# Attention output kept transposed in SBUF through the attention stage and stored to DRAM after the last loads

## The reference

```python
# attention over memory slots, per batch and head (b = h = 8, s = 576, d = 64, m = 32)
a = softmax(phi, axis=s); k_m = einsum('bhsm,bhsd->bhmd', a, k); v_m = einsum('bhsm,bhsd->bhmd', a, v)
attn = softmax(q @ k_m.T / sqrt(d)) @ v_m
x = attn reshaped to (4608, 512)
# first layer: w_in (512, 2048), w_out (2048, 512)
h = x @ w_in; x = (h * sigmoid(1.702 * h)) @ w_out
# mixture of 8 experts, the top one of each token: w1[e] (512, 1024), w2[e] (1024, 512)
out = gate_weight * output_gate * (relu(x @ w1[e]) @ w2[e])
```

## Time and profile before

| | us |
|---|---|
| three runs | 1408.29, 1414.30, 1414.38 |
| median | 1414.3 |
| the profiled execution's own time | 1402.57 |
| its span in the profile | 1400.9 |
| mean granted clock of TensorE | 0.993 |

### The profile page before, as it was taken

The page is one execution under the profiler, slowest core; times in us unless marked ns, Lnnn a source line. Parts: engine busy times, 40 slices in busy tenths (PEclk is TensorE's granted clock), DMA queues, the critical chain, the costliest instruction groups (busy, mean ns, idle before and its releaser), DMA issues.

```text
span 1400.9 us, 26210 instructions
## 1 busy us (share of the span) xinstructions
PE 1351.8 (96%) x7922; PEld 1094.9 (78%) x7923; DVE 681.5 (49%) x1400; ACT 403.2 (29%) x725; POOL 517.7 (37%) x612
## 2 busy tenths in 40 slices
PE   5888899999999999999999999999999999999997
PEld 4566688888888888888888888887788888888885
DVE  4789633344353343433534344436655555555553
ACT  2455422222232232222322223223332222223221
POOL 1100486345443343433433334331434333433331
PEclk9999999999999999999999999999999999999999
DMA  9999635656556556465465654665784688649882
GB/s 229 290 325 313 234 100 168 194 200 194 181 191 183 179 169 182 171 187 175 160 183 176 179 192 147 184 189 203 236 257 119 164 254 249 185 115 261 246 237 61
DMA packets 164843, 275.31 MB, mean 197 GB/s; under 512 B 20179, under 2 KB 57316, under 8 KB 164788
## 3 DMA queue, kind: packets, MB, share of 16 engines
q1 hardware_dynamic: 104260, 197.16, 44.7%
q10 hardware_dynamic: 47408, 45.63, 12.7%
q0 software_dynamic: 13120, 31.82, 7.3%
HBM read 146.03 MB, written 100.45 MB: 176 GB/s over the span
## 4 chain that ended last, share of the span: by engine, by line
PE 86%; DVE 5%; DMA 3%; issue 3%; SPq 2%; ACT 0%; ACTq 0%; POOL 0%; DVEq 0%; POOLq 0%
PE ps L672 28%; PE ps L706 28%; PE ps L776 14%; PE ps L747 14%; DMA ph<-in_phi 1%; PE ps L716 1%; DMA qraw<-in_q 1%; SPq L426 1%; SPq L454 1%; PE ps L649 1%; DVE cmeta L1123 1%; DVE phT L1101 1%; DMA cq<-ch 1%; PE ps L631 0%; DMA cmeta<-record_scratch 0%
## 5 line engine op out<-in xcount | busy, mean ns | idle before, releaser
L672 PE MATMUL ps<-xs,W 128*128 (+1 forms) x1728 | 417.6, 391 | 1.1 <-DVE xs L1162 1.1
L706 PE MATMUL ps<-W,gs 128*128 128x512 f32 x1728 | 415.3, 390 | 0.1
L672 PEld LDWEIGHTS ps<-xs,W 128*128 128x128 f32 x1728 | 323.1, 188 | 72.0 <-issue 4.1
L706 PEld LDWEIGHTS ps<-W,gs 128*128 128x128 f32 x1728 | 324.3, 188 | 68.1 <-DVE gs L1217 0.8
L1215 DVE TENSOR_TENSOR gate<-ps,gate 128x512 f32<-128x512 f32 x144 | 99.6, 691 | 364.0 <-ACT gate L932 363.7
L932 ACT ACTIVATE gate<-ps 128x512 f32<-128x512 f32 x144 | 86.2, 598 | 471.3 <-PE ps L672 470.8
L776 PE MATMUL ps<-W,chT 128*128 (+1 forms) x936 | 218.3, 390 | 1.2 <-DVE chT L1348 1.2
L747 PE MATMUL ps<-W,cx 128*128 (+1 forms) x936 | 218.5, 390 | 0.5 <-issue 0.5
L1540 POOL CAST whi<-raw 128x512 fp32r<-128x512 f32 x128 | 81.3, 635 | 337.9 <-DMA raw<-in_moe_w 337.9
L776 PEld LDWEIGHTS ps<-W,chT 128*128 128x128 f32 x936 | 175.6, 188 | 38.3 <-issue 2.0
L747 PEld LDWEIGHTS ps<-W,cx 128*128 128x128 f32 x936 | 175.6, 188 | 37.3 <-issue 1.1
(11 more groups left out here) (158 smaller groups left out, 891.1 us busy)
## 6 DMA issues: line engine op xcount, KB each, us to landing
W<-expert_scratch SPq DMA_DIRECT2D x24, 2048.0 KB, 11.7
raw<-in_moe_w SPq DMA_DIRECT2D x128, 256.0 KB, 2.8
expert_scratch<-whi SPq DMA_DIRECT2D x128, 256.0 KB, 2.6
expert_scratch<-raw SPq DMA_DIRECT2D x128, 256.0 KB, 2.9
cq<-ch ACTq DMA_DIRECT2D x156, 128.0 KB, 3.9
crec<-record_scratch POOLq DMA_DIRECT2D x160, 64.0 KB, 5.6
kvm<-in_k SPq DMA_DIRECT2D x32, 288.0 KB, 5.2
kvm<-in_v SPq DMA_DIRECT2D x32, 288.0 KB, 7.0
```

Of the source, the lines that this page charges most:

```text
L672: mm = pe.matmul(ps[:, f % 2, :], W[:, col:col + P], xs[:, bass.ds(x0 + (x_lo * K1 + c) * T, T)], start=(c == 0 and w_lo + x_lo == 0), sto ...
L706: mm = pe.matmul(ps[:, 2 + s, :], gs[:, f % 2, g_lo, s * P:(s + 1) * P], W[:, col:col + DM], start=(f == 0 and g_lo + w_lo == 0), stop=(f ...
```

## The change

The tensor `xk` lies over the part of W where W_out and the second half of W_in come later. It has room for all 16 groups, in reverse order, so `xo` goes. `x_out` copies into it and issues nothing. The stores are made in five lots (`STORES`), each with its own semaphore:

- SP, after the last q load of attention: groups 0 and 1, then 8 and 7; then it waits for groups 0 and 1 to have landed before `load_x(0)` and the first two weight chunks of the layer.
- ScalarE: groups 6 and 5 at the end of group 14; 4, 3 and 2 at the end of group 15; 13, 12, 14 and 15 after `g_step(0, 1)`; 11, 10 and 9 after `g_step(0, 2)`.
- GpSimd waits for lots before it splits a chunk into their place: lots 0 and 1 before chunk 4, lot 2 (6, 5, 4, 3, 2) before chunk 12, lot 3 (13, 12, 14, 15) before chunk 13, lot 4 (11, 10, 9) before chunk 21. SP waits for lot 2 before `load_x(1)`.

ScalarE's wait for all stores moves from step 2 of tile 0 to step 15, VectorE's is dropped. `groups` loops over groups 3 to 10 in two passes and writes out groups 11 to 15.

```diff
+        STORES = ((0, 1), (8, 7), (6, 5, 4, 3, 2), (13, 12, 14, 15), (11, 10, 9))
+            sbt(a, "before_xk", [P, SLOT // 2])
+            xk = sbt(a, "xk", [P, NG * 2 * S])
-            xo = sbt(a, "xo", [P, 2, 2, S])
+        def kept(g):
+            return xk[:, bass.ds((NG - 1 - g) * 2 * S, 2 * S)].rearrange("p (a n) -> p a n", a=2)
+        def store_x(eng, i, groups):
+            for g in groups:
+                eng.dma_start(xT_dram[2 * (g % 2) * P:(2 * (g % 2) + 2) * P, g // 2 * S:(g // 2 + 1) * S].rearrange("(a p) n -> p a n", a=2),
+                              kept(g)).then_inc(s_xst[i], 16)
+        def stored_x(eng, i):
+            eng.wait_ge(s_xst[i], 16 * len(STORES[i]))
...
-            with eng.Fori(0, (NG - 4) // 4) as m:
+            with eng.Fori(0, (NG - 8) // 4) as m:
...
-            body(NG - 1, B - 1, 3)
+            for g in range(NG - 5, NG):
+                body(g, g // 2, g % 4)
...
-            for i in range(2):
-                sp.wait_ge(s_xst[i], 16)
+            sp.wait_ge(s_xo, 2 * 9)
+            store_x(sp, 0, STORES[0])
+            store_x(sp, 1, STORES[1])
+            stored_x(sp, 0)
             load_x(0)
...
                         if k == 1:
+                            stored_x(sp, 2)
                             load_x(t + 1)
...
-                if i == 0:
-                    wait(act, s_xst[u], 16 * b)
-                act.copy(xo[:, u, :, i * HS:(i + 1) * HS], ps[:, bank:bank + 2, 0:HS]).then_inc(s_xo, 1)
-                if i == 1:
-                    wait(act, s_xo, 2 * g + 2)
-                    act.dma_start(xT_dram[2 * u * P:(2 * u + 2) * P, bass.ds(b * S, S)].rearrange("(a p) n -> p a n", a=2),
-                                  xo[:, u]).then_inc(s_xst[u], 16)
+                act.copy(kept(g)[:, :, i * HS:(i + 1) * HS], ps[:, bank:bank + 2, 0:HS]).then_inc(s_xo, 1)
...
+                if isinstance(g, int) and g == NG - 2:
+                    act.wait_ge(s_xo, 2 * 7)
+                    store_x(act, 2, STORES[2][:2])
+                if last:
+                    store_x(act, 2, STORES[2][2:])
...
+                    if first and f == 1:
+                        act.wait_ge(s_xo, 2 * NG)
+                        store_x(act, 3, STORES[3])
                     if first and f == 2:
+                        store_x(act, 4, STORES[4])
+                    if first and f == STEPS - 1:
                         stage_a_done(act)
...
-                    if first and f == 2:
-                        stage_a_done(dve)
...
+                            if f in (0, 4):
+                                stored_x(pool, 1 if f == 0 else 2)
+                            if f == 0:
+                                stored_x(pool, 0)
                             split_w(K1 + 2 * f, 0, SLOT + f * CH)
+                            if k > 1 and c == 0:
+                                stored_x(pool, k + 1)
                             split_w_in(K1 + 2 * f + 1, c, k)
```

More of the change, by code:

```diff
@@ L120, in build @@
         sb("to_512", [P, 96 - RING * (NE + 4)])
+        with ExitStack() as a:
+            sbt(a, "before_xk", [P, SLOT // 2])
+            xk = sbt(a, "xk", [P, NG * 2 * S])
         W = sb("W", [P, 2 * SLOT], F32R)
@@ L250, in build @@
         s_xo = sem("attn_out_copied")
-        s_xst = [sem(f"xT_stored{i}") for i in range(2)]
+        s_xst = [sem(f"xT_stored{i}") for i in range(len(STORES))]
         s_passed = {e.engine: sem(n) for e, n in ((nc.vector, "vector_waits_passed"), (nc.gpsimd, "pool_waits_passed"),
@@ L314, in build @@
         block = ctx.enter_context(nc.Block())
+        def kept(g):
[6 more added lines that the diff above has]
+            eng.wait_ge(s_xst[i], 16 * len(STORES[i]))
         def stage_a_done(eng):
-            for i in range(2):
-                eng.wait_ge(s_xst[i], 16 * B)
+            for i in range(len(STORES)):
+                stored_x(eng, i)
         STEPS = C1
@@ L877, in q_out, with x_out @@
                     act.copy(q_flat[:, 512:QA * D], ps[:, 2:4, :].rearrange("p k n -> p (k n)")[:, 512 - P:]).then_inc(s_qT, 1)
-            def x_out(g, b, u, i, bank=4):
+            def x_out(g, i, bank=4):
                 wait(act, s_o, 2 * g + i + 1)
-                if i == 0:
-                    wait(act, s_xst[u], 16 * b)
-                act.copy(xo[:, u, :, i * HS:(i + 1) * HS], ps[:, bank:bank + 2, 0:HS]).then_inc(s_xo, 1)
-                if i == 1:
-                    wait(act, s_xo, 2 * g + 2)
-                    act.dma_start(xT_dram[2 * u * P:(2 * u + 2) * P, bass.ds(b * S, S)].rearrange("(a p) n -> p a n", a=2),
-                                  xo[:, u]).then_inc(s_xst[u], 16)
+                act.copy(kept(g)[:, :, i * HS:(i + 1) * HS], ps[:, bank:bank + 2, 0:HS]).then_inc(s_xo, 1)
             def x_hi(t, c):
@@ L912, in group @@
                 if not isinstance(g, int) or g >= 2:
-                    x_out(g - 2, b - 1, u, 0)
+                    x_out(g - 2, 0)
                 q_out(g, 1)
@@ L918, in group @@
                 if not isinstance(g, int) or g >= 2:
-                    x_out(g - 2, b - 1, u, 1)
+                    x_out(g - 2, 1)
+                if isinstance(g, int) and g == NG - 2:
[3 more added lines that the diff above has]
+                    store_x(act, 2, STORES[2][2:])
             exp_phi(0, 0)
             groups(act, group)
-            x_out(NG - 2, B - 1, 0, 0)
+            x_out(NG - 2, 0)
             exp_scores(NG - 1)
-            x_out(NG - 2, B - 1, 0, 1, 2)
+            x_out(NG - 2, 1, 2)
             def g_step(t, f):
@@ L1034, in _ @@
             g_step(0, 0)
-            x_out(NG - 1, B - 1, 1, 0, 6)
-            x_out(NG - 1, B - 1, 1, 1)
+            x_out(NG - 1, 0, 6)
+            x_out(NG - 1, 1)
             tiles(act, act_tile)
```

## The result

The change made the kernel slower: 20 runs of it gave 1420.6 us at the median (1413.6 to 1430.7), 20 runs of the kernel before 1407.8 us (1402.2 to 1414.4). The ratio is 1.0092, interval 1.0072 to 1.0111. The forecast was a ratio of 0.9972 (1410.4 against 1414.3) and a range that ended at 1417.5. The three runs known at the time had lain at the upper end of what the kernel before does, which hid part of the distance. The profiled execution of the changed kernel took 1416.7 us, its span is 1415.0 us, 14.1 us more than before.

A forecast was written before the change was run, and what follows sets the result against it. TensorE bounds the kernel from the first layer on, so attention counts by when the layer starts; transfers pace groups 2 to 6, VectorE later ones. Terms -4.8 + 0 + 0.9 + 0 = -3.9 us gave 1410.4 us, range 1404.5 to 1417.5.

The forecast's parts named there:

- Stores out of the loop: Attention, groups 2 to 6: without stores, loads keep up from group 4 on; -4.8 us, bounds 0 and 5.2.
- Four groups written out: End of attention: group 15's 1.35 us stop moves to group 11, no further stops; 0, bounds 0 to 5.4 us.
- Tile 0 of x: Before the first layer: x's load behind four stores lands 0.8 us early to 1.9 late; cost 0.9 us, at most 12.7 late.
- Stores in tile 0: First layer: the lot before chunk 13 lands 2.3 us late, within 4.1 us of cover; cost 0.
- Issues and moved waits: ScalarE's store issues (0.38 us each) are hidden or covered, and moved waits come after the stores should have landed; 0.
- Rival 3: Start of layer: tile 0 of x arrives behind the stores, making it slower; likely 1420 us, up to 1426; chance 0.1.
- Rival 1: Attention and layer start: the gain is given back (4.8 saved, 4.8 lost) or never came (0 saved); 1414 us; chance 0.2.

The follow-up runs named there:

- Experiment 2: Kernel before, with every attention store of x issued twice, the second into an unread scratch tensor; ratio 1.0053 to the kernel before.
- Experiment 1: Kernel before, with only the loop shortened: groups 11 to 15 written out, two passes instead of three, stores untouched; ratio 1.0044 to the kernel before.
- experiment 3: Changed kernel, with SP storing groups 0 and 1 ahead of the loads of groups 13 and 14; ratio 1.0044 to the kernel before.
- experiment 6: Changed kernel, with the loop of the kernel before and groups 0 and 1 stored ahead of the loads of groups 13 and 14; ratio 1.0020 to before.
- experiment 8: experiment 7 with x's tile 0 loaded ahead of the stores of 8 and 7, and 6 and 5 stored after group 15's copies; ratio 0.9992 to before.
- experiment 7: experiment 6 with x's tile 1 loaded after the third weight-chunk lot, and the last store lot at step 5 instead of 2; ratio 1.0018 to before.
- Experiment 4: Changed kernel, with tile 1 of x loaded after the third lot of weight chunks, behind chunk 19 instead of 11; ratio 1.0071 to the kernel before.
- experiment 10: experiment 8 with stores spread more: 4, 3, 2 after group 14's last copy, 13 and 12 at step 1, 14 and 15 at step 2; ratio 1.0017 to before.
- experiment 5: Changed kernel, with the loop of the kernel before (only group 15 written out) and groups 6 and 5 stored at group 15's start; ratio 1.0041 to before.
- experiment 9: Kernel before, with q loads issued from GpSimd's queue instead of SP's, stores still in the loop; ratio 1.0001 to the kernel before.

## Why the prediction was wrong

The sum had M, the start of the layer, 3.9 us earlier; it came 7.9 us later (161.07 against 153.13), and 6.2 us more were lost behind it.

- **Stores out of the loop, -4.8 us: wrong, groups 2 to 10 gained 0.2 us.** (The 1.0 us up to group 2 lies almost wholly before the first store of the kernel before, so it is not the change's.) The failed step is "less than one store costs at either rate. So without stores the loads should keep up from group 4 on". It priced a store at its bytes over a rate, and took that for time that the loads would get back. Experiment 2 and the bytes of three kernels show that beside these loads a store costs nearly nothing up to a total of 351 GB/s (40 to 80 us); 1.1 us a group came at 366 GB/s, where VectorE had set the pace. The term's lower bound (the loads alone hold the stage) was right; the prediction had its evidence in hand, the 11.4 us period without stores, and the 240 GB/s row, whose low rate it read as a higher price for a store, where it was the loads' own ceiling. At that rate a group's 2.06 MB take 8.6 us, over the 7.99 us that the sum gave each group, and the two were never set side by side.
- **Four groups written out, 0: wrong, up to 0.4% of the time.** The first half held: the stop after the loop moved to group 11 (1.34 us). "Groups 1 and 2 ... run without such a stop, so I take 0" failed: groups 12 and 13 have one each as well, of up to 2.91 us, over the bound of 1.35. Experiment 1 shows the whole effect alone. Straight-line code stops three times in a row, at places that move by 16 or 17 matmuls a group, beside the extra transfers of instructions. The Trainium skill's page "Runtime: NRT & Kernel Launch", section "Instruction fetch mechanics", says that instructions are fetched ahead in sequence and that a taken branch breaks this; that the four groups cost nothing by it is contradicted by the 0.44% of experiment 1. That the fetch queues behind the full DMA engines is likely, and was not tried by itself.
- **Tile 0 of x, +0.9 us: wrong by far, the wait is 8.45 us.** From the first load of group 15 to the use of x it took 156.91 - 133.95 = 23.0 us where the sum said 14.5. x was wanted 14.5 us after that load, much as assumed. The failed step is "Through the DMA engines go, in order": it added bytes as if x's load stood in the queue right behind the stores. But SP can issue it only once groups 0 and 1 have landed, and those land beside 8 and 7. So there are two full trips in series, 10.06 and 8.43 us in the chain, instead of 5.5 + 2.4 + 1.5. The upper bound (x 12.7 us late) held it. The rate was low for part of it: 228 GB/s from 138 to 143 us, beside the last loads, where the sum priced the stores at 430; from 143 to 155 us it was 400 to 410. The engines were full all through (share 1.01 from 138 to 148 us), so how the 8.45 us split between the series, what shared the engines, and the low rate is not known. Experiments 3, 6 and 8 take parts away: groups 0 and 1 landing late, then what stood ahead of x or beside it. The Trainium skill's page "DMA: Bandwidth & Descriptors", section "Queues, rings and completion order", says that a completion lands only after all earlier writes of that DMA engine; whether it does so here stays undecided. In experiment 7 x lands after 16.0 us at the end of a stretch at 400 GB/s, last of all by that rule and by the bytes alike.
- **The clock: left out.** Having let TensorE run dry costs time on top of the waits: 1.5 us in the first `mm1`, 1.3 us in `mm1(0, 8)`.
- **Stores in tile 0, 0: wrong, 2.9 us and its clock.** It watched the lot before chunk 13, but the chunk that came late is 12, behind tile 1 of x; "Behind SP's wait stands chunk 12, with the cover above" named the place and gave it the cover that the other delay had to use too. Stores and chunks were only added up for one of them. Experiment 4 shows one part, the place of tile 1 of x. The rest is not settled: a wait of about 2 us for chunks is left in experiments 4, 8 and 10 and is absent in 6 and 7.
- **Issues and moved waits, 0: held in time, not in size.** Seven stores took ScalarE 6.76 us to issue where the sum had 7 x 0.38 = 2.7, but TensorE waited for nothing but GpSimd in `mm1` (2.9 us in all), and 0.1 us in `mm2`.
- **Rival 3 was what happened**, with its place and near its likely size (1420). That the size fits is in part luck: of the 7.9 us by which M moved, 2.8 come from groups 10 to 14, which it did not hold, and its stores at 240 GB/s were true for the first 5 us only. Rival 1's "0 saved" was true as well. The two together, with the written-out groups, go beyond each.

Shares by the runs: written-out groups 0.4 to 0.5% (experiments 1 and 5), the wait for groups 0 and 1 to land some 0.5% (experiment 3), both together 0.7% (6), the places of x and of the stores around it and in tile 0 the remaining 0.2% (7 and 8). Each has an interval of about a quarter of a per cent either way, so the last is not told from nothing.

## What to carry to other kernels

Before pricing a removed transfer at its bytes, compare the rate of the remaining ones in a stretch where it is absent: if they run no faster there, its removal returns nothing. When a load has to wait for a store's landing, count two full trips and all that shares the engines, and issue it ahead of whatever does not need to go first. Where a loop is written out while the DMA engines are full, count a stop for each written-out copy: 1.2 to 3.4 us in three of four groups here.

## What was not expected of the hardware

- These loads (rows of k, v, q and phi) run at 229 to 246 GB/s from 40 to 80 us with all 16 engines near full by their share, from one queue or two, with or without stores; stores added 59 to 120 GB/s on top. What holds the loads (the time of their packets in the engines or the reads in DRAM) stays open.
- Issuing a store is not a fixed price: 0.38 us each before, in the changed kernel 3.19 us for four and 3.57 us for three, with the engines full.
- A stop of 1.77 us came in group 6 of the changed kernel, in the first pass of the loop. Stops of 0.7 to 2.0 us stand in the same pass in experiments 3, 4, 6, 8 and 10 and in 9, which keeps the stores in the loop (1.51 us), but not in the kernel before. A transfer of instructions begins at 66 us in the changed kernel and in the kernel before alike, so it does not decide by itself. The cause is open.
- In experiment 8 the clock fell to the lower level at the start of the layer with no wait for x before it: granted 0.60 from 154 to 158 us, the first `mm1` 4.60 us, after a stretch in which TensorE was busy 1.01 of 2 us. In experiment 10 the same stretch was followed by 3.06 us. It is not known what decided.
